# Sparse attention with two chained MLPs on one core: the start of the first chunk reordered, three units opened on three of their four source blocks, gate copies issued one bank read earlier, and the last joins given to VectorE

## The reference, cut to what matters

```python
# q, k, v: (4, 8, 576, 64)
scores = scale * np.matmul(q, k.transpose(0, 1, 3, 2))
kth = np.partition(scores, -32, axis=-1)[..., -32:-31]
scores = np.where(scores >= kth, scores, -1000000000.0)
attn = np.exp(scores - np.max(scores, axis=-1, keepdims=True))
attn = attn / (np.sum(attn, axis=-1, keepdims=True) + 1e-09)
x = np.matmul(attn, v)                  # then as 2304 tokens x 512
h = x @ w_in                            # first MLP, 512 -> 2048
x = np.maximum(0.01 * h, h) @ w_out
h = x @ w_in2                           # second MLP
g = np.where(h >= 1, h, np.where(h <= -1, 0.0, (h + 1) ** 2 / 4))
return g @ w_out2
```

## Time and profile before

| | |
|---|---|
| time, median of 3 runs | 1240.78 us (1239.79 to 1243.62) |
| the profiled execution | 1243.76 us |
| its span in the profile | 1241.7 us |
| PE matmuls busy | 1125.9 us (91%) |
| DVE busy | 892.0 us (72%) |
| ACT busy | 701.0 us (56%) |
| POOL busy | 641.0 us (52%) |

### The profile page before, as it was taken

How to read it: one execution, slowest core, us unless ns; L and a number is a source line. 1 busy time by engine, 2 the same in 40 slices (tenths; PEclk the granted TensorE clock), 3 DMA queues, 4 the chain that set the end, 5 groups by cost and what they waited for, 6 DMA issues and landing times.

```text
span 1241.7 us, 21057 instructions
## 1 busy us (share of the span) xinstructions
PE 1125.9 (91%) x7360; PEld 1013.0 (82%) x7360; DVE 892.0 (72%) x2056; ACT 701.0 (56%) x1577; POOL 641.0 (52%) x614
## 2 busy tenths in 40 slices
PE   3545998969999999999999989999899999999998
PEld 2333987859888789888987878898789998999997
DVE  7999978989889989899989978969999001100111
ACT  5655777656667756676666655666765424322231
POOL 5665768735446634555545553445754326422343
PEclk9856999889999999999999979999999999999999
DMA  6786998856665677777676646545455677787763
GB/s 220 281 311 231 344 342 299 279 175 196 221 242 204 220 271 269 259 245 248 226 237 206 245 146 223 178 163 183 136 187 200 210 244 237 260 272 247 248 235 110
DMA packets 86504, 287.12 MB, mean 231 GB/s; under 512 B 9600, under 2 KB 13184, under 8 KB 86400
## 3 DMA queue, kind: packets, MB, share of 16 engines
q1 hardware_dynamic: 78912, 270.04, 63.1%
q10 hardware_dynamic: 7488, 15.73, 3.7%
HBM read 247.46 MB, written 38.27 MB: 230 GB/s over the span
## 4 chain that ended last, share of the span: by engine, by line
PE 63%; DVE 13%; POOL 9%; ACT 8%; issue 4%; DMA 2%; ACTq 0%; POOLq 0%; SPq 0%
PE ps_f L738 17%; PE ps_f L740 15%; PE ps_f L739 15%; PE ps_av L701 7%; DVE top L950 5%; POOL gate L581 5%; DVE work L953 4%; PE ps_s L657 2%; PE ps_t L678 2%; DVE part_r L977 2%; POOL drop L566 2%; PE ps_t L684 2%; ACT gate L879 1%; PE ps_t L657 1%; ACT part_r L868 1%
## 5 line engine op out<-in xcount | busy, mean ns | idle before, releaser
L738 PE MATMUL ps_f<-gate,w_ring 128*128 128x384 f32 (+2 forms) x896 | 293.5, 328 | 29.6 <-POOL gate L581 29.5
L950 DVE MAX8 top<-work 128x8 f32<-128x576 f32 x432 | 309.0, 741 | 0.1
L738 PE MATMUL ps_f<-xy,w_ring 128*128 128x384 f32 (+2 forms) x896 | 289.9, 324 | 11.4 <-POOL xy L591 7.6
L566 POOL TENSOR_TENSOR drop<-scores,drop 128x576 f32<-128x576 f32 x144 | 207.3, 1440 | 156.8 <-DVE drop L959 156.8
L739 PE MATMUL ps_f<-gate,w_ring 128*128 128x384 f32 (+2 forms) x896 | 284.3, 317 | 0.0
L740 PE MATMUL ps_f<-gate,w_ring 128*128 128x384 f32 (+2 forms) x896 | 284.2, 317 | 0.0
L740 PE MATMUL ps_f<-xy,w_ring 128*128 128x384 f32 (+2 forms) x896 | 281.0, 314 | 0.0
L739 PE MATMUL ps_f<-xy,w_ring 128*128 128x384 f32 (+2 forms) x896 | 280.9, 314 | 0.0
L738 PEld LDWEIGHTS ps_f<-gate,w_ring 128*128 128x128 f32 x896 | 173.6, 194 | 49.1 <-POOL gate L581 33.2
L953 DVE MATCH_REPLACE8 work<-top,work 128x576 f32<-128x576 f32 x288 | 212.5, 738 | 0.0
L738 PEld LDWEIGHTS ps_f<-xy,w_ring 128*128 128x128 f32 x896 | 170.5, 190 | 29.3 <-issue 14.5
(11 more groups left out here) (87 smaller groups left out, 1830.8 us busy)
## 6 DMA issues: line engine op xcount, KB each, us to landing
w_ring<-w_split SPq DMA_DIRECT2D x412, 512.0 KB, 4.1
w_split<-w_ring SPq DMA_DIRECT2D x36, 512.0 KB, 5.9
raw<-wd SPq DMA_DIRECT2D x64, 256.0 KB, 5.0
w_split<-xy SPq DMA_DIRECT2D x28, 512.0 KB, 3.7
kq<-kqd ACTq DMA_DIRECT2D x12, 576.0 KB, 5.9
v_sb<-vd ACTq DMA_DIRECT2D x12, 320.0 KB, 3.9
kq<-kqd SPq DMA_DIRECT2D x4, 576.0 KB, 7.1
out_t<-y_acc ACTq DMA_DIRECT2D x12, 192.0 KB, 4.3
```

What stands on the lines that cost most here:

```text
L566: pool.tensor_tensor(slot, scores[:, it.n % S_SLOTS, t - it.first, :], slot, ALU.add).then_inc(masked, 1)
L738: pe.matmul(out, w[:, 0, m], high, start=b == 0, stop=False)
L950: dve.max(top[:, t % T_SLOTS, 8 * r:8 * r + 8], source(t, r)).then_inc(dve_step, 1)
```

## The change

1. The head, ACT, steps up to 21. `copy_transposed` of an item stands one step later, behind that step's exponential, except for the last item of chunk 0, which is copied at once in step 21 ahead of the exponential. `copy_values` stands behind the weight pieces of its step. On POOL `low_x` comes one step later. The scores of item 11 are computed in step 20, not 21.
2. The head, DVE. The sum of chunk 0's last item is closed ahead of the fourth `drop8` of its tile.
3. The head, PE. In step 21, ahead of the last item's transposes, the first three units open their banks and run over source blocks 0 to 2 (nine matmuls each). In step 22 each of them runs over the fourth block alone. Each block has its own wait.
4. The plan of chunk 0: in steps 22 to 43 a step is filled with `FIRST_FILL` = 4142.5 instead of 4350, so that its 48 units reach into step 43. All steps from 44 on have the same units as before.
5. ACT's `event` finishes unit u - 2 ahead of the read of unit u, everywhere.
6. In the tail DVE joins behind its own curve (`tail_joined`) for the 32 hidden units of layer 2 there, and POOL no longer joins them.

```diff
+FIRST_NS = 2 * BLOCKS * PRODUCTS * (BLOCK_F * CK + CK * BLOCK_F) * (CHUNKS[0].width / 2.4 + 12)
+FIRST_FILL = FIRST_NS / (READY[1] - READY[0])
...
-    if it.first <= 20:
-        return max(0, it.first - 2)
+    if it.first < READY[0]:
+        return max(0, it.first - 2, ITEMS[it.n - S_SLOTS].last + EXP_LAG if it.n >= S_SLOTS else 0)
...
-        credit += FILL
+        credit += FILL if s >= READY[1] else FIRST_FILL
...
+TAIL = min(n for n, s in STEP_OF_UNIT.items() if s == ATTENTION_STEPS)
+EARLY_UNITS = UNITS[:BANKS]
... POOL
-                    to_join.append(u)
+                    if u.n < TAIL:
+                        to_join.append(u)
-                if s - 1 in VALUES_AT and s < READY[0]:
-                    low_x(VALUES_AT[s - 1])
+                if s - 2 in VALUES_AT and s < READY[0]:
+                    low_x(VALUES_AT[s - 2])
... PE
-                if u.hidden and u.i == 0 and not u.layer and not u.block:
-                    pe.wait_ge(x_low_done, u.chunk.last_gp + 1)
+                        if not u.layer and not u.block and u.i == 0:
+                            pe.wait_ge(x_low_done, u.chunk.last_gp - CK + 1 + b + 1)
...
             def feed(u):
+                if u.n < len(EARLY_UNITS):
+                    products(u, [CK - 1])
+                    return
                 open_bank(u)
...
+                if s == READY[0] - 1:
+                    for u in EARLY_UNITS:
+                        open_bank(u)
+                        products(u, range(CK - 1))
                 if s in OUT_AT:
                     transpose(OUT_AT[s])
... ACT
             def event(u):
-                read_bank(u)
                 if to_finish and to_finish[0].n <= u.n - FINISH_LAG:
                     finish(to_finish.pop(0))
+                read_bank(u)
...
                 if done and s < READY[0]:
                     normalise(done)
+                if awaited:
+                    copy_transposed(done)
                 if s < READY[0] and 0 <= s - EXP_LAG:
                     exponential(s - EXP_LAG)
+                if s - 1 in OUT_AT and s < READY[0]:
+                    copy_transposed(OUT_AT[s - 1])
... DVE
+                    if u.n >= TAIL:
+                        dve.wait_ge(curved, u.in_layer + 1)
+                        over = part_o[:, u.h % G_SLOTS, 0:u.width]
+                        dve.tensor_tensor(over, r, over, ALU.add).then_inc(tail_joined, 1)
...
+                if soon:
+                    close_sum(shut)
+                    count += 1
                 if new:
                     dve.wait_ge(dve_step, second_top)
                     drop8(t, 1)
```

More of the change, by code:

```diff
@@ L177 @@
 FILL = 4350.0
+PRODUCTS = 3
 def starts_early(gp):
@@ L291 @@
 STEP_OF_UNIT = {u.n: s for s, groups in enumerate(PLAN) for g in groups for u in g}
+TAIL = min(n for n, s in STEP_OF_UNIT.items() if s == ATTENTION_STEPS)
+TAIL_HIDDEN = min(u.in_layer for u in HIDDEN if u.layer and u.n >= TAIL)
+EARLY_UNITS = UNITS[:BANKS]
 def next_needs(u):
@@ L343, in scores_first @@
     return s in OUT_AT
-SCORED_EARLY = sum(score_step(it) < READY[0] for it in ITEMS)
+SCORED_EARLY = sum(score_step(it) < READY[0] - 1 for it in ITEMS)
 ITEMS_OUT = [sum(out_step(o) < score_step(it) for o in ITEMS) for it in ITEMS]
@@ L437, in build @@
         joined = sem("joined")
+        tail_joined = sem("tail_joined")
         gate_high_done = sem("gate_high_done")
@@ L877, in finish @@
                 if u.hidden:
-                    act.wait_ge(joined, u.in_layer + 1)
+                    if u.n < TAIL:
+                        act.wait_ge(joined, u.in_layer + 1)
+                    else:
+                        act.wait_ge(tail_joined, u.in_layer - TAIL_HIDDEN + 1)
                     act.activation(gate[:, 0, u.slot, 0:u.width], part_o[:, u.h % G_SLOTS, 0:u.width],
@@ L905, in _ @@
                     copy_values(CHUNKS[0].last_gp)
+                awaited = done and done.last == LAST_OF_GROUP[CHUNKS[0].last_gp]
                 if done and s < READY[0]:
                     normalise(done)
+                if awaited:
+                    copy_transposed(done)
                 if s < READY[0] and 0 <= s - EXP_LAG:
                     exponential(s - EXP_LAG)
+                if s - 1 in OUT_AT and s < READY[0]:
+                    copy_transposed(OUT_AT[s - 1])
                 if scores_first(s) or s < READY[0]:
@@ L914, in _ @@
                     exponential(s - EXP_LAG)
[L915 to L918, removed]
                 for a in direct_pieces(s):
@@ L922, in _ @@
                     high_piece(i)
+                if s - 1 in VALUES_AT and s < READY[0]:
+                    copy_values(VALUES_AT[s - 1])
                 for u in first:
@@ L1027, in _ @@
                     last_top = count
+                soon = shut and shut.last == LAST_OF_GROUP[CHUNKS[0].last_gp]
+                if soon:
+                    close_sum(shut)
+                    count += 1
                 if new:
@@ L1031, in _ @@
                     count += 1
+                if soon:
+                    dve.wait_ge(dve_step, count - 1)
+                    invert_sum(shut)
                 for u in third:
                     event(u)
-                if shut:
+                if shut and not soon:
                     close_sum(shut)
```

## The result

The changed kernel takes 1221.68 us (median of 4 runs, 1219.97 to 1223.14), the kernel before 1242.20 on the same chip: ratio 0.9835, 95% interval 0.9809 to 0.9861, 20.5 us less. 1223.7 (1212 to 1234) had been predicted. The profiled execution took 1223.14 us, its span is 1221.2.

A forecast was written before the change was run, and what follows sets the result against it. DVE's search paces the head, PE and DVE are level in chunk 0, PE alone bounds the tail. Gains of 7.2 + 2.5 + 2 + 5.4 = 17.1 us take the median 1240.78 to 1223.7 us, range 1212 to 1234.

The forecast's parts named there:

- Start of chunk 0: Head into chunk 0: fourth unit starts on PE at 120.2 instead of 127.41, 7.2 us gained; gains of 2 to 9.3 possible.
- 27 matmuls moved are the most: Start of chunk 0: moved matmuls give most of the 7.2 us, the warm array in transposes and products 3.3.
- DVE's waits for exponentials: Head: DVE's stalls for exponentials on ACT fall from 4.7 to about 1 us; not yet on PE's path.
- Rest of chunk 0: Filled step 43: an output unit of 2.9 us lands where PE idled, 2.5 us gained; bounds 4.6 lost, 8.6 gained.
- Finish ahead of read: 280 to 985 us: ACT's waits for low gates go, gates come earlier to PE; 2 us gained, bounds 14.6 gained, 19 lost.
- ACT at joins: 280 to 985 us: ACT waits at the join of a unit just read, delaying work queued behind; up to 19 us lost.
- many waits at joins: Sign of a wrong prediction: ACT's gate copies wait many times for joins between 280 and 985 us.
- Tail: Tail: PE sets the pace, layer 2 reads about 2.1 us apart instead of 2.46; 5.4 us gained, bounds 0 and 6.3.
- The bound of 6.3: Tail: upper bound of the gain, equal to all of PE's waits there for low gates, 6.3 us.
- The head's gain is given back: Rival, chance 0.22: PE meets DVE or a missing weight piece; about 2 of 7.2 + 2.5 us stay, 1231 us.
- More goes than I count: Rival, chance 0.13: half of PE's 8.6 and 14.6 us of gate waits go, plus the filled step; 1214 us.
- The port: Rival, chance 0.10: DVE and POOL block each other in the tail, period stays 2.46 us, tail gives nothing; 1229 us.

The follow-up runs named there:

- e8: Kernel before with only gate copies ahead of reads and tail joins on DVE; head, early matmuls and plan as before: 1226.60 us.
- e11: The changed kernel itself, unedited, timed again in more rounds: 1220.18 us.
- e3: Changed kernel without early matmuls: the 27 matmuls stand behind the products with v again; 1218.18 us.
- e7: Changed kernel without early matmuls, and the first unit waits for all of x ahead of its first block: 1221.82 us.
- e6: Changed kernel without early matmuls and with the old order of ACT and POOL in the head: 1225.46 us.
- e4: Changed kernel with steps 22 to 43 filled with 4350 ns again, so step 43 holds no unit: 1218.48 us.
- e5: Changed kernel without early matmuls and with steps 22 to 43 filled with 4350 ns again: 1217.96 us.
- e1: Changed kernel with ACT reading unit u ahead of finishing unit u - 2 everywhere, as before the change; tail joins stay on DVE: 1234.55 us.
- e2: Changed kernel with POOL joining again in the tail and DVE only making curves; finish stays ahead of read: 1223.76 us.

## Why the prediction was right, step by step

The total was right (17.1 forecast, 20.5 measured) by luck as much as by reasoning: an excess in the first half and a shortfall in the second offset each other. Start and rest of chunk 0 were put at 9.7 us, the order and the tail at 7.4. By e8 the order and the tail are 16.5, and parts 1 to 4 on top of them bring 4.9 (6.4 by e11).

- *Start of chunk 0, 7.2 us.* At the fourth unit it is 6.6, with the block 1.4 us later than taken and 1.3 us shorter, since the clock stood at 2.4 GHz. The step that failed is "27 matmuls moved are the most". Without them (e3) 4.8 of the 6.6 us are still there. Counted from item 7's transposes, the early matmuls are 2.8, the block-by-block wait 1.3 (e7), ACT's order 2.4 (e6 to e3). And 2.8 us there weren't 2.8 us at the end. A small slip in the working changed nothing: the rows put the end of the scaling at 110.9 (110.46 + 1.43 - 1), not 110.6, which takes the bound of 9.3 to 9.0.
- *DVE's waits for exponentials* fell to 4.3, not 1 us. The step failed; nothing on PE's path hung on it.
- *Rest of chunk 0, 2.5 us.* The step "lands where PE idled" failed. Step 44 starts at 273.32 instead of 279.24, 5.9 us, less than the start had gained. The stretch did get its work: from 262 us to step 44 PE is busy without a break, where it had idled 4.5 of the 18 us from 262 to 280 before. But e4 and e5 show the kernel no slower with the old fill, and from the fourth unit to tile 42 the old fill is about 1 us shorter in both pairs.
- *Finish ahead of read, 2 us.* The mechanism was right, the size was off: 6.1 us between tiles 42 and 143 (668.6 to 662.5), 7.6 by e1 against the changed kernel. PE's idle time between the two marks fell by 5.8 us (26.3 to 20.6), so this gain is waiting taken away. For chunk 0 there was no term; e8 ends it 3.2 us earlier, but e1 contradicts the order as the reason. What I set against it, ACT at joins, grew by 10.5 us and reached PE nowhere that a mark shows. I had named many waits at joins as a sign of being wrong; they came, 17 instead of 1, and cost nothing visible, so the sign was a bad one.
- *Tail, 5.4 us.* The reads are 2.08 us apart as forecast and the gate waits went from 6.3 to 0.9, exactly 5.4. It gained 8.6. Of the rest, 1.7 us are the clock: behind the last stalls before, PE ran at 0.50 and 0.66 of full speed in the windows 1224 to 1226 and 1226 to 1228, and at 1.00 in the changed kernel behind its last one. Another 1.5 I can't place. The bound of 6.3 was too low, for half of the excess because it counted the waits and not what follows them. The windows before:

```profile
1224.00:1226.00 2.00, 1.91 (x6) 1.91 (x7) 0.55 (x1) 0.00 (x0) 0.04 (x1) 0.50 0.00 0
1226.00:1228.00 2.00, 2.00 (x10) 2.00 (x9) 0.01 (x1) 0.00 (x0) 0.00 (x0) 0.66 0.26 98
```

- *The rivals.* "The head's gain is given back" came true in part, with more time at 1.2 GHz and not by DVE or a transfer. "More goes than I count" did not come as told: PE's waits for gates went from 14.6 to 10.5 us in the middle, not to half, and in chunk 0 from 8.6 to 9.2. The port blocks each join, as its rival said, without lengthening the period.

Left open: why the changed program, in three profiled executions out of three (with e2 and e11), stays at 1.2 GHz 6.8 us longer behind the same stalls than e3. That this goes with the loss is shown by the marks; what sets its length isn't.

## What to carry to other kernels

Follow the loop that sets a period link by link, and ask of each edit whether it is in the loop: here the order of copy and read was, the join was not, and moving the join to an engine that carries another stage cost 16 us where it was busy. A gain at one place counts only where the next mark still has it; undo each part by itself before crediting it. When a stage stalls on the last result of a block, try one more independent unit ahead of the consumers: here it gave 4.8 us, more than the join moved to DVE in the tail.

## What the runs showed of the hardware

The stalls of 1 to 2.6 us at the end of chunk 0 were followed by 6.8 to 13.7 us at 1.2 GHz, also when PE was busy again. So removing a stall can give more than its length: the tail gained 8.6 us from 5.4 us of waits, and 1.7 of the other 3.2 are matmuls no longer at half clock. And a kernel that wins 2.8 us early can lose them by more time of this kind: the same program had 20.5 us of it between the fourth unit and tile 42 in three executions out of three, and without the early matmuls it had 10.2 and was 5.2 us shorter there.
